# Two score levels of a linear-attention kernel computed in tiles of the TensorE array

## The reference

```
for t in range(S):                       # S = 768, per batch and head
    cur   = (u * k[t]) outer v[t]
    y[t]  = r[t] @ (state + cur)
    state = w[t][:, None] * state + k[t] outer v[t]
```

## Time and profile before

| | |
|---|---|
| median of three timed runs | 498.38 us (497.99 to 499.42) |
| span of the profiled execution | 495.7 us |
| timed median less that span | 2.7 us |
| PE busy, share of the span | 453.0 us, 91% |
| DVE busy | 304.8 us, 61% |
| ACT busy | 182.5 us, 37% |
| POOL busy | 201.1 us, 41% |
| mean granted clock of TensorE | 0.996 |

### The profile page before, as it was taken

The page is one execution under the profiler, slowest core; times in us unless marked ns, Lnnn a source line. Parts: engine busy times, 40 slices in busy tenths (PEclk is TensorE's granted clock), DMA queues, the critical chain, the costliest instruction groups (busy, mean ns, idle before and its releaser), DMA issues.

```text
span 495.7 us, 8582 instructions
## 1 busy us (share of the span) xinstructions
PE 453.0 (91%) x2936; PEld 438.5 (88%) x2936; DVE 304.8 (61%) x490; ACT 182.5 (37%) x350; POOL 201.1 (41%) x212
## 2 busy tenths in 40 slices
PE   1898798798888789989999999999999999999997
PEld 1798787788788789879999999999989999989997
DVE  4897898898897477855232232141158957389572
ACT  3766666657553242111111211121136612167220
POOL 2986867767766776844850000000010701006000
PEclk9999999999999899999999999999999999999999
DMA  8942602602500182695600000000000000200002
GB/s 296 391 190 97 252 10 95 223 39 95 198 0 0 42 340 65 201 327 216 217 25 0 0 0 0 0 1 1 1 0 2 0 1 15 82 3 0 1 0 95
DMA packets 8678, 43.64 MB, mean 88 GB/s; under 512 B 1104, under 2 KB 3024, under 8 KB 6864
## 3 DMA queue, kind: packets, MB, share of 16 engines
q1 hardware_dynamic: 7648, 30.36, 17.2%
q0 software_dynamic: 1008, 12.99, 6.8%
HBM read 40.99 MB, written 2.36 MB: 87 GB/s over the span
## 4 chain that ended last, share of the span: by engine, by line
PE 56%; DVE 1%; issue 0%; ACT 0%; ACTq 0%; DVEq 0%
PE PS L939 18%; PE PS L937 18%; PE PS L938 18%; PE PS L1059 1%; PE PS L1047 1%; DVE ME L767 1%; DVE BN L761 0%; DVE HL L807 0%; DVE OUT L924 0%; DVE X L759 0%; ACT HH L589 0%; DVE BN L772 0%; DVE MV L763 0%; ACTq L597 0%; DVEq L766 0%
## 5 line engine op out<-in xcount | busy, mean ns | idle before, releaser
L959 PE MATMUL PS<-RM,KW 128*128 128x128 f32 x672 | 86.3, 286 | 24.6 <-DVE KW L675 13.0
L959 PEld LDWEIGHTS PS<-RM,KW 128*128 128x128 f32 x672 | 80.8, 197 | 29.6 <-issue 18.5
L807 DVE SCALAR_TENSOR_TENSOR HL<-PS,HH 128x384 fp32r<-128x384 f32 x48 | 26.6, 557 | 95.8 <-ACT HH L589 95.6
L589 ACT ACTIVATE HH<-PS 128x384 fp32r<-128x384 f32 x48 | 23.4, 492 | 119.3 <-PE PS L939 111.8
L463 POOL COPY XB<-X 128x384 f32<-128x384 f32 x12 | 6.2, 538 | 145.8 <-PE PS L1059 145.8
L500 ACT COPY RM<-RW 64x384 f32<-64x384 f32 x96 | 49.6, 516 | 24.0 <-PE PS L959 12.4
L682 DVE COPY_PREDICATED AT<-MASK,PS 128x768 f32<-128x768 int32 x40 | 53.8, 1345 | 0.0
L386 POOL TENSOR_TENSOR RW<-RW,WP 128x384 f32<-128x384 f32 x48 | 45.9, 967 | 14.0 <-ACT RM L500 14.0
L937 PE MATMUL PS<-W2H,HH 128*128 128x384 f32 x144 | 48.5, 337 | 2.2 <-DVE HL L807 2.2
L937 PE MATMUL PS<-UTH,W1H 128*128 128x384 f32 x144 | 48.5, 336 | 0.6 <-DVE UTL L790 0.6
L939 PE MATMUL PS<-W2H,HL 128*128 128x384 f32 x144 | 48.1, 334 | 0.0
(11 more groups left out here) (134 smaller groups left out, 1053.8 us busy)
## 6 DMA issues: line engine op xcount, KB each, us to landing
STG<-rkw_dram SPq DMA_DIRECT2D x8, 1152.0 KB, 7.2
RKT<-rk_dram SPq DMA_DIRECT2D x4, 1152.0 KB, 5.4
RAW<-w_dram SPq DMA_DIRECT2D x6, 768.0 KB, 4.4
VST<-v_dram SPq DMA_DIRECT2D x4, 864.0 KB, 4.5
W1H<-w_dram POOLq DMA_DIRECT2D x1, 2304.0 KB, 9.5
W2H<-w_dram POOLq DMA_DIRECT2D x1, 2304.0 KB, 14.4
SGH<-w_sgt_dram POOLq DMA_DIRECT2D x1, 2304.0 KB, 11.6
RAW<-w_sgt_dram SPq DMA_DIRECT2D x3, 768.0 KB, 4.3
```

The source lines that it names most:

```text
L589: act.activation(HH[:, f % HSLOT, :], PS[:, 2 + f % 3, 0:TC], ACT.Relu).then_inc(s_hh, 1)
L807: dve.scalar_tensor_tensor(HL[:, f % HSLOT, :], PS[:, 2 + f % 3, 0:TC], 0.0, HH[:, f % HSLOT, :].bitcast(F32), ALU.max, ALU.subtract).then ...
L959: last = pe.matmul(scores(lev, j)[:, c * C:(c + 1) * C], KW[:, j, c * C:(c + 1) * C], RM[:, j, lev % 2, c, :, :], start=True, stop=True)
```

## The change

Level 5 is computed in halves. A chunk of 128 tokens holds two pairs of blocks of 32, and scores between the two halves of the chunk are not wanted; so the left 64 tokens of `KW` meet only the left 32 right-block columns of each head. Two matmuls of 64 weight columns and 64 moving columns, one for each half, write partitions 0 to 63 and 64 to 127 (two column tiles of the array). Level 6 is computed for each head alone: 64 partitions of `KW` and of `RW` (two row tiles), 64 left tokens as weights, 64 right tokens moving, read from `RW` itself. So level 6 needs no `RM`, and ACT's four copies for it go. POOL's update of `RW` at level 6 now waits for the scores of that step in place of the copy, and PE waits for POOL's update of level 5. The moves to `AT` read other places of PSUM, as many elements as before. PE's loop over the four iterations is written out, with constants as wait values.

```diff
@@ -48,6 +48,9 @@
 ORIGIN, ROOM = 16512, 212832
 
 
+MASKED_RM = NLEV - 1
+
+
 TABLE = 2 * TT * (NK + HALF // 2) + KD * D
 
 
@@ -247,6 +250,14 @@
 
 
 
+        def half_scores(j):
+
+            return PS[:, 4 + 2 * j, 0:NC * C // 2].rearrange("p (c a n) -> p c a n", c=NC, a=2)
+
+        def head_scores(j):
+
+            return PS[0:C // 2, 2 * j:2 * j + 2, 0:NC * C // 2].rearrange("p a (c n) -> p a c n", c=NC)
+
         y_banks = (slice(1, 4, 2), slice(4, 6))
 
         def x_at(b, t, n=1, col=0, width=D):
@@ -319,7 +330,7 @@
 
                 sp.wait_ge(s_copied, i * 4 + 4 + START)
                 sp.wait_ge(s_upr, i * (2 * NLEV) + 2 + START)
-                sp.wait_ge(s_rm, i * (4 * NLEV) + 4 + START)
+                sp.wait_ge(s_rm, i * (4 * MASKED_RM) + 4 + START)
                 sp.wait_ge(s_upk, i * (2 * NLEV) + 2 + START)
                 sp.wait_ge(s_wp, i * (2 * NLEV) + 2 + START)
                 load_rkw(i * 2 + 2)
@@ -378,9 +389,12 @@
                         decay = STG[:, j, 2, :] if lev == 0 else WP[:, j, wbase(lev):wbase(lev) + S // length]
                         if lev == 0:
                             pool.wait_ge(s_copied, i * 4 + (3 + j) + START)
+                        elif lev == NLEV - 1:
+                            pool.wait_ge(s_upr, step - 1 + START)
+                            pool.wait_ge(s_scores, step + 1 + START)
                         else:
                             pool.wait_ge(s_upr, step - 1 + START)
-                            pool.wait_ge(s_rm, i * (4 * NLEV) + 4 * lev + 2 * j + 2 + START)
+                            pool.wait_ge(s_rm, i * (4 * MASKED_RM) + 4 * lev + 2 * j + 2 + START)
                         right = split(RW[:, j, :], length)[:, :, 1, :]
                         left_decay = decay.rearrange("p (m two) -> p m two", two=2)[:, :, 0:1]
                         pool.tensor_tensor(right, right, left_decay.broadcast_to([P, S // length // 2, length]),
@@ -520,11 +534,13 @@
                     act.wait_ge(s_y, i * 2 + (j - 1) + START)
 
                     act.wait_ge(s_picked, i * (2 * MASKED) + (2 * MASKED - 1 + j) + START)
-                    for m in range(C // length // 2):
-                        rows = slice(2 * m * length, (2 * m + 1) * length)
-                        act.copy(AT[rows, j, :, :, (2 * m + 1) * length:(2 * m + 2) * length].rearrange("p c a l -> p (c a) l"),
-                                 scores(lev, j)[rows, :].rearrange("p (q m l) -> p q m l", q=2 * NC, l=length)[:, :, m, :]
-                                 ).then_inc(s_moved, 1)
+                    if lev == NLEV - 1:
+                        act.copy(AT[0:length, j, :, :, length:C].rearrange("p c a l -> p a c l"), head_scores(j)).then_inc(s_moved, 1)
+                    else:
+                        for m in range(2):
+                            rows = slice(2 * m * length, (2 * m + 1) * length)
+                            act.copy(AT[rows, j, :, :, (2 * m + 1) * length:(2 * m + 2) * length],
+                                     half_scores(j)[rows, :, :, :]).then_inc(s_moved, 1)
 
                 for lev in range(1, NLEV):
                     for j in range(2):
@@ -532,7 +548,8 @@
                         act.wait_ge(s_upr, step - 1 + START)
                         if lev >= 2:
                             act.wait_ge(s_scores, step - 3 + START)
-                        right_blocks(i, lev, j)
+                        if lev < MASKED_RM:
+                            right_blocks(i, lev, j)
                         if lev == MASKED + 1:
                             move(MASKED, j)
                 move(NLEV - 1, 0)
@@ -938,11 +955,14 @@
                 pe.matmul(dst, lh, rl, start=False, stop=False)
                 return pe.matmul(dst, ll, rh, start=False, stop=stop)
 
-            with pe.Fori(0, NIT) as i:
+            for i in range(NIT):
                 for lev in range(NLEV):
                     for j in range(2):
                         step = i * (2 * NLEV) + (2 * lev + j)
-                        pe.wait_ge(s_rm, i * (4 * NLEV) + 4 * lev + 2 * j + 2 + START)
+                        if lev == NLEV - 1:
+                            pe.wait_ge(s_upr, step - 1 + START)
+                        else:
+                            pe.wait_ge(s_rm, i * (4 * MASKED_RM) + 4 * lev + 2 * j + 2 + START)
                         if lev == 0:
                             pe.wait_ge(s_copied, i * 4 + (j + 1) + START)
                             pe.wait_ge(s_kvm, i * 2 + START)
@@ -954,10 +974,21 @@
                             pe.wait_ge(s_x, i * 2 + START)
                         if lev >= 2:
                             pe.wait_ge(s_picked, i * (2 * MASKED) + (2 * (lev - 2) + j + 1) + START)
+                        half = C // 2
                         for c in range(NC):
-
-                            last = pe.matmul(scores(lev, j)[:, c * C:(c + 1) * C], KW[:, j, c * C:(c + 1) * C],
-                                             RM[:, j, lev % 2, c, :, :], start=True, stop=True)
+                            if lev < MASKED:
+                                last = pe.matmul(scores(lev, j)[:, c * C:(c + 1) * C], KW[:, j, c * C:(c + 1) * C],
+                                                 RM[:, j, lev % 2, c, :, :], start=True, stop=True)
+                            elif lev == MASKED:
+                                for b in range(2):
+                                    last = pe.matmul(half_scores(j)[b * half:(b + 1) * half, c, :, :],
+                                                     KW[:, j, c * C + b * half:c * C + (b + 1) * half],
+                                                     RM[:, j, lev % 2, c, :, b * half // 2:(b + 1) * half // 2], start=True, stop=True)
+                            else:
+                                for a in range(2):
+                                    rows = slice(HOLD * a, HOLD * (a + 1))
+                                    last = pe.matmul(head_scores(j)[:, a, c, :], KW[rows, j, c * C:c * C + half],
+                                                     RW[rows, j, c * C + half:(c + 1) * C], start=True, stop=True)
                         last.then_inc(s_scores, 1)
                 for j in range(2):
                     at = 4 + 2 * j
```

## The result

The changed kernel takes 509.23 us (median of 4 runs, 508.63 to 510.03) against 498.9 of the kernel before in the same runs: a ratio of 1.0216, 95% interval 1.0192 to 1.0239. The forecast was 503 and the range ended at 509.0, so the direction was right and the size was not.

A forecast was written before the change was run, and what follows sets the result against it. No engine is full; a cross-engine chain bounds each iteration, PE's with no time to spare, POOL's with 0.49 us. POOL's wait +3.2, loop -0.8, clock +2.4 give +4.8 on 498.38: 503 us; 8-in-10 range 497.2 to 509.

The forecast's parts named there:

- Ladder steps on PE: Level 5 and 6 steps go from 12 records to 24 smaller ones; 1.1 us a step, bounds 0.72, 1.44 and 2.7.
- POOL's update waits for scores: POOL's level 6 update waits for step (6, 1), delaying L392, both L396 and y: 0.8 us an iteration, +3.2 over four.
- my own bound with 0.72: With ladder steps of 0.72 us, POOL's L396 ends near 117.05 and the loss is 0.35 an iteration, +1.4.
- Turns of DVE and POOL: Two-input DVE and POOL instructions do not run together: KW updates take 1.68 and 1.75 against 0.53; L396 without turn 1.27.
- The loop written out: PE's attention loop as constants saves 0.07 us a wait, two or three waits an iteration: -0.8 over four, bounds 0 and -2.8.
- Clock of TensorE: PE's 3.3 us gap ahead of y lowers the clock in two of four iterations, 1.2 us each: +2.4, bounds 0 and 6.8.
- the bound of 1.7: Price of one clock fall in the y block if TensorE ran at exactly half speed: 1.7 us, against 1.2 taken.
- The clock's upper bound: Clock falls in all four y blocks at 1.7 us each: 6.8 us.
- Every sign that I had named for a right forecast: Profile signs: wait over 2 us, POOL after step (6, 1), L410 0.9 to 1.9 later, clock 0.5 in y, steps 0.8 to 1.5.

The follow-up runs named there:

- e4: The changed kernel with POOL's two level 6 updates of RW put behind the three instructions on RKT: 497.63 us, ratio 0.9959 to the kernel before.
- e1: The kernel before with PE's attention loop written out and nothing else: 497.65 us, ratio 0.9983.
- e13: The changed kernel with 6 useless matmuls an iteration ahead of PE's wait for SBD: 503.1, 505.7 and 508.4 us, ratio 1.0131, leaving out a fourth run of 579.4.
- e6: The kernel before, without tiles, with two more POOL multiplications in each iteration to make its POOL chain longer: 514.83 us, ratio 1.0336.
- e7: The changed kernel with POOL's level 6 updates put behind one RKT instruction (the second L406) alone: 504.28 us, ratio 1.0122 to the kernel before.
- e8: The changed kernel with DVE's two reduces to DSB put behind the SBD work: 492.26 us, ratio 0.9865 to the kernel before.

## Why the prediction went wrong

- **Ladder steps on PE.** I took 1.1 us between bounds of 0.72 and 1.44. Measured 0.70 (24 records in 0.92, less the 0.22 of the last one): the low bound. The Trainium skill, TensorEngine Tiling (Array Packing), Tiling Modes, Key Properties, had said that tiles load and multiply in parallel, and the trace agrees. Of the drain at a change of mode that it also names the trace shows nothing: L984 follows L980 at 71.33 with no idle time, L999 follows L990 at 76.00, within 0.05 us. (The mode changes at three places of an iteration, not at the four that I counted.)
- **POOL's update waits for scores.** The mechanism was right: y waits for POOL's products in every iteration, both L716 run without a pause, PE's chain is faster to no use. The size was smaller: L410 ends 81.73 - 52.73 = 29.0 us after the ladder's start, 0.9 later than before and not 1.3, and y starts 0.15 to 0.2 later in three iterations and 0.55 in the fourth, not 0.8; that is 1.1 in all, the loop written out included, against +3.2 - 0.8. Of the difference in an iteration 0.45 is the step's length (my own bound with 0.72 was 0.35 us late); the rest is that the `SBD` work behind it had a little more spare time than I had read: two L716 in a row take 1.21 us, not 2 x 0.66.
- **Turns of DVE and POOL.** They held: L410 takes 1.38 when DVE is idle (I had worked out 1.27), 1.72 when it takes turns, and they undid most of the expected gain of e4. I had written this down and then left it out of e4's sum.
- **The loop written out.** -0.8 forecast. The trace of e1 shows -0.3 (an iteration of 38.03 in place of 38.1); more than that can't be told from the times.
- **Clock of TensorE. This is the step that failed.** I had the wait right (3.3 us forecast, 3.06 measured) and put +2.4 us on it: a fall in two of four iterations, 1.2 us each. Measured: a fall in all four, 2.6 us each, 10.4 us of 11.5 in the span. Three things were mis-sized. I took the length of the low stretch from the only example, 3.4 us; here it was 6.8. Why it is the one or the other is not shown: e13 has both with the same code and the same wait. I took the pace from a stretch with matmuls cut at both edges: 12 records counted in 2.00 us are fewer than 12 whole ones. The half pace was in the trace before, as the bound of 1.7 said. And I took two of four for want of a second example, though the wait was longer than the one that had sufficed. There was a second one, which I overlooked: the 2.24 us at 215.65, without a fall.
- With 4 x 2.6 in place of 2.4 for the clock and 1.1 in place of 3.2 - 0.8 my own sum gives 498.4 + 1.1 + 10.4 = 509.9, against 509.23 measured. The clock's upper bound, 4 x 1.7 = 6.8, was too small as well, by the stretch of 3.4. Every sign that I had named for a right forecast was there (the wait over 2 us, POOL's order of events, L410 0.9 later, the clock at 0.5 in the y block, 24 records in 0.92 us), so the mechanism was right, and its largest term came out at a quarter of its size. That the end of the range, 509.0, lay so near the measured time is luck: POOL's term was too large where the clock's was too small.

## What to carry to other kernels

A wait ahead of a block that is all TensorE costs twice: its own length, and the lower clock in the block behind it; price the second at half of the low stretch that lies in the block, with both lengths seen here (3.4 and 6.8 us), and with a fall every time as the upper bound. The length of the wait alone did not tell whether the clock would fall. A faster step in a ladder moves the path to whatever stands behind the next engine in program order: here it stood behind two reduces that nobody needed yet. In this kernel it paid to move the consumer that waits, and not the producer: POOL's products moved forward collided with the updates that set the pace.

## What the runs showed of the hardware

- No length of wait parted falls of the clock from none. Ahead of y it fell after waits of 3.06 us (four of four), 2.13 to 2.15 (e6, four of four), 1.72 to 1.74 (e13, three of four) and 1.69 to 1.71 (e7, three of three). In the MLP PE waits 2.10 to 2.74 us for DVE, and the clock fell there in 5 of the 13 profiled executions, after 2.27 to 2.53, and not after 2.24, 2.60, 2.63 or 2.74. In e4 it fell twice where PE had waited 0.72 and 1.08 us.
- Once down it stayed for some 3.4 us or for some 6.8, in every trace of this case; in the y block of the changed kernel PE was busy for the last 5.5 of the 6.8.
- A low clock cost time only where PE set the pace: 2.5 to 2.7 us in a y block of the changed kernel, nothing in the ladder of e4.
- At the lower level fp32 records of 96 columns stand 0.214 us apart in place of 0.112. That is a factor of 1.9, near the 2 between the two levels, 1.2 and 2.4 GHz.
- Matmuls of 64 weight and 64 moving columns in fp32 cost 0.029 us a record in two tiles, a quarter of the 0.120 of full ones, with 64 or with 128 partitions.
- While a POOL product runs, a DVE instruction with both inputs in SBUF is held up (the first L722 of e8, 0.98 in place of 0.31 us), and one that reads PSUM is not (L710, 0.66).
